# First batch of attention: the mask reads the scores in PSUM, against a threshold in the scores' own sign and scale

## The chip, the cores and the metric

The kernel runs on one core of a Trainium2 chip. The metric is the time of one execution on the device in microseconds, lower is better; the median of several runs counts. Everything is float32 (matmul operands are float32 split into a rounded high part and a low rest). Engines are named as in the profile: PE is TensorE (PEld its weight loads), DVE VectorE, ACT ScalarE, POOL GpSimd, SP the queue that issues most DMAs.

## The reference

Three stages follow one another. Attention keeps, in every row of scores, only those within `tau` of the row's maximum. Then come a gated two-layer block, and a block with a Fourier transform and an MLP.

```python
scores = scale * np.matmul(q, k.transpose(0, 1, 3, 2))      # scale = 1/sqrt(64), 4 batches x 8 heads, 576 x 576
thresh = np.max(scores, axis=-1, keepdims=True) - tau
scores = np.where(scores >= thresh, scores, -1000000000.0)
scores = scores - np.max(scores, axis=-1, keepdims=True)
attn = np.exp(scores)
attn = attn / (np.sum(attn, axis=-1, keepdims=True) + 1e-09)
out = np.matmul(attn, v)
...
xk = mu_k * x + (1.0 - mu_k) * x_prev                       # and xr with mu_r
k = np.maximum(xk @ w_k, 0.0)
v = k * k @ w_v
r = 1.0 / (1.0 + np.exp(-(xr @ w_r)))
x = r * v
...
u = x + np.real(np.fft.fft(np.fft.fft(x, axis=1), axis=2))
un = (u - mu) / np.sqrt(var + 1e-06)
ch = np.maximum(un @ w_ch1, 0.0) @ w_ch2
y = u + ch
```

## The kernel before

**Tiles.** Attention goes in tiles of 128 queries by all 576 keys. The heads of a batch are taken in pairs. A pair has nine tiles (`TILES_PAIR`): four of the first head, the tail tile (`TAIL`, the fifth, number 4 of the pair) that holds the last 64 queries of both heads, and four of the second head. A batch has four pairs, so 36 tiles (`TILES_BATCH`), and all four batches 144 (`TILES`). Tiles are numbered n = 0 to 143.

**The steps of a tile**, each on its engine:
- PE, `qk(n)` (L863): the scores into PSUM, two halves of 288 keys in two banks, by four matmuls (`k_hi` and `k_lo` for each half); a tail tile takes eight. In the first batch the tile has the two-bank tensor `PB[n % 2]`. From tile 36 on all tiles have `PB[0]`, since `PB[1]` then serves the dense stages.
- DVE, `row_max(n)` (L1414): reads the scores in PSUM, multiplies them by `taus[:, 2:3]` (minus the scale), writes the negated scaled scores to `neg_s` in SBUF, and gives their minimum, `negmax`. It announces `max_ready`.
- ACT, `exp(n)` (L1146, L1147): the threshold `negmax + |tau|`, a 128 x 1 operation, and `exps`, the exponential of the whole tile out of `neg_s`.
- DVE, `mask(n)` (L1429): `probs = (neg_s <= thresh) * exps` with the row's sum; in a tail tile one more operation for the last 64 keys (`both_last`, L1428). It announces `probs_ready`. After the tail tile and the last tile of a pair come two small operations for the inverse sums.
- PE, `transpose_probs(n)` (L881), four or five transposes in two units; ACT, `copy_units(n)` (L1156), copies the two units to `probsT`; PE, `pv(n)` (L901, L903), eight or nine pieces of the product with the values.
- ACT, `copy_tile` (L1174, L1177): the finished outputs, scaled, to `x_att`.

**The order** is written out by hand. Every engine walks over slots n = 0, 1, 2, ... and takes in slot n:
- PE: `qk(n)`, `transpose_probs(n-3)`, `pv(n-4)`, then dense work due in this slot.
- DVE: `row_max(n)`, `mask(n-1)`, then dense work.
- ACT: `exp(n)`, in slots 9 to 35 also a rounding of weights or tables (`weight_hi`), dense work, `copy_units(n-2)`, `copy_tile`.
- POOL: the low parts of the next keys and queries (`split_step`: L671, L685, L692) and of the weights and tables (L696 to L713), then dense work.

In the first batch there is no dense work yet. Dense work on a batch begins when its attention is done: in slot 38 for the first one. Semaphores order the engines; a buffer is given back by a semaphore too. The score buffer is given back for `qk(n)` by the wait that the change touches:

```python
if n >= TILES_BATCH:
    pe.wait_ge(max_ready, n)
elif n >= 2:
    pe.wait_ge(max_ready, n - 1)
```

so in the first batch `qk(n)` waits until the row maxima of tiles 0 to n-2 are done. `row_max(n)` for its part waits for `probs_ready` of tile n-2, since it overwrites the `neg_s` buffer that `mask(n-2)` read.

Of the kernel before, what the change touches and what calls it, by code (L numbers as in the profile page):

```python
# [22 lines left out]
F32 = mybir.dt.float32  # L23
F32R = mybir.dt.float32r
ALU = mybir.AluOpType
# [7 lines left out]
P128 = 128  # L33
# [35 lines left out]
EPS_SM = 1e-9  # L69

# [16 lines left out]
def place_of(n):  # L87


    return (2, 2, 1, 1, 0, 0, 0, 1, 1)[n % TILES_PAIR] * DH  # L90

# [140 lines left out]
def build(nc, qT, kT, v, tau, mu_k, mu_r, w_k, w_v, w_r, w_1, w_2, dft_d, dft_odd, dft_s, ident_in, cd_scr, odd_scr, cs_scr, u_scr, out):  # L232
    ctx = ExitStack()
    with ctx:
# [25 lines left out]
        taus = m.put("taus", [P128, 4], F32)  # L260
# [256 lines left out]
        with nc.Block() as block:  # L517
# [316 lines left out]
            def _(pe):  # L834
# [5 lines left out]
                def qk(n):  # L840
# [10 lines left out]
                    if n >= TILES_BATCH:  # L851

                        pe.wait_ge(max_ready, n)
                    elif n >= 2:
                        pe.wait_ge(max_ready, n - 1)
# [118 lines left out]
                def dense(d):  # L974

                    for dt in range(DT):
                        yield x_at(d, dt)
                        wait_evicted(d, "x", 0, dt)
                        if dt == 0 and d == 0:
                            pe.wait_ge(max_ready, TILES_BATCH)  # L980
# [158 lines left out]
            def _(act):  # L1139
                def exp(n):  # L1140
                    act.wait_ge(max_ready, n + 1)
                    if n >= 2:

                        act.wait_ge(probs_ready, n - 1)
                    col = n % (2 * TILES_PAIR)
                    nc.scalar.activation(thresh[:, col:col + 1], negmax[:, col:col + 1], ACT.Identity, bias=taus[:, 1:2]).then_inc(thr_ready, 1)  # L1146
                    nc.scalar.activation(exps[:, n % 2, :], neg_s[:, n % 2, :], ACT.Exp,  # L1147
                                         bias=negmax[:, col:col + 1], scale=-1.0).then_inc(exp_ready, 1)
# [202 lines left out]
                act.wait_ge(setup_b, 1)  # L1351
# [35 lines left out]
            def _(dve):  # L1387
# [16 lines left out]
                dve.wait_ge(setup_b, 1)  # L1404
                dve.wait_ge(pool_ready, 1)
# [11 lines left out]
                def mask(n):  # L1417
# [7 lines left out]
                    if jj == TAIL:  # L1425

                        twice = [t[:, n % 2, FULL * P128:S].unsqueeze(1).broadcast_to([P128, 2, DH]) for t in (neg_s, exps)]
                        nc.vector.scalar_tensor_tensor(both_last[:, :, :], twice[0], thresh[:, col:col + 1], twice[1], ALU.is_le, ALU.mult)  # L1428
                    nc.vector.scalar_tensor_tensor(probs[:, n % 2, place_of(n):place_of(n) + S], neg_s[:, n % 2, :], thresh[:, col:col + 1],  # L1429
                                                   exps[:, n % 2, :], ALU.is_le, ALU.mult,  # L1430
                                                   accum_out=rowsum[:, jj, 0:1]).then_inc(probs_ready, 1)
# [318 lines left out]
```

## Time and profile before

| | |
|---|---|
| runs, median | 1062.2 us (3 runs, 1061.6 to 1063.57) |
| the profiled execution, its own time | 1061.17 us |
| its span, first to last instruction | 1059.4 us |
| PE busy | 1032.3 us, 97% of the span |
| DVE busy | 584.9 us, 55% |
| ACT busy | 502.3 us, 47% |
| POOL busy | 415.4 us, 39% |
| granted TensorE clock, mean | 0.998 of full speed |

A busy share over the whole span is a mean over stages of different kinds: attention alone (about the first 100 us), attention beside dense work of the batch before, and the MLP at the end. So the tables by stretch of time and the timeline are read beside it. In a timeline row the bracket at the end tells how long the engine had stood idle before and who released it. An instruction that also writes an accumulator is followed by a row `DVE_READ_ACCUMULATOR`; its end is what others wait for.

### The profile page before, as it was taken

Reading aid. Unit: us, or ns where it says so; the run is one execution under the profiler, and the core shown is the slowest. Engines: PE = TensorE matmul, PEld = TensorE weight load, DVE = VectorE, ACT = ScalarE, POOL = GpSimd, SP = SyncE. Lnnn points to the kernel's source line nnn. Section 1 sums busy time; section 2 is a strip of 40 time slices with the busy share of each in tenths; the row PEclk is TensorE's granted clock in tenths of the full one; section 3 lists DMA queues with packets and bytes.
Section 4 is the critical chain, followed back from the end, with each engine's and each line's share of the span. In section 5 each row is a group of like instructions: output and inputs, shape, how many; then the busy total and the mean of one; then the engine's idle time right before and its main releaser. Section 6 shows DMA issues by size and latency. Waiting matters only on the chain.

```text
span 1059.4 us, 18202 instructions
## 1 busy us (share of the span) xinstructions
PE 1032.3 (97%) x6896; PEld 980.2 (93%) x6896; DVE 584.9 (55%) x1135; ACT 502.3 (47%) x1252; POOL 415.4 (39%) x363
## 2 busy tenths in 40 slices
PE   6999899999999999999999999999999999999998
PEld 5898899999999999999999999888888888888998
DVE  6998995467975477874565687443214214114111
ACT  5989785656775646775646643211111111111110
POOL 5878784333664434673423246331211211111000
PEclk9999999999999999999999999999999999999999
DMA  8736112033302032301023137101001100100000
GB/s 241 200 89 193 43 44 58 3 91 118 103 26 59 1 126 83 104 25 37 20 94 111 45 121 278 41 1 63 10 1 37 36 1 34 39 1 1 37 1 35
DMA packets 41271, 70.08 MB, mean 66 GB/s; under 512 B 6624, under 2 KB 22368, under 8 KB 40672
## 3 DMA queue, kind: packets, MB, share of 16 engines
q1 hardware_dynamic: 40880, 68.59, 20.6%
q8 instruction: 55, 0.90, 0.4%
q10 hardware_dynamic: 304, 0.33, 0.1%
q14 instruction: 32, 0.26, 0.1%
HBM read 56.50 MB, written 12.41 MB: 65 GB/s over the span
## 4 chain that ended last, share of the span: by engine, by line
PE 86%; DVE 4%; POOL 3%; ACT 3%; issue 3%; DMA 0%; SPq 0%; DVEq 0%; ACTq 0%; POOLq 0%
PE PB L836 22%; PE PB L837 21%; PE PB L838 21%; PE PB L901 8%; PE PB L863 6%; PE PB L881 5%; DVE probs L1429 2%; PE PB L903 1%; ACT probsT L1156 1%; ACT exps L1147 1%; PE PB L986 1%; DVE neg_s L1414 1%; POOL k_lo L692 0%; POOL q_hl L685 0%; POOL cs_lo L713 0%
## 5 line engine op out<-in xcount | busy, mean ns | idle before, releaser
L1373 ACT ACTIVATE h_hi<-PB 128x464 fp32r<-128x464 f32 (+1 forms) x80 | 44.4, 554 | 329.9 <-PE PB L838 329.9
L1652 DVE SCALAR_TENSOR_TENSOR h_lo<-PB,h_hi 128x464 fp32r<-128x464 f32 (+1 forms) x80 | 51.0, 637 | 256.7 <-ACT h_hi L1373 256.7
L1429 DVE SCALAR_TENSOR_TENSOR probs<-neg_s,thresh,exps 128x576 f32<-128x576 f32 x144 | 160.7, 1116 | 0.5 <-ACT exps L1147 0.2
L901 PE MATMUL PB<-v_sb,probsT 128*128 128x64 f32 (+1 forms) x1152 | 146.1, 270 | 0.0
L901 PEld LDWEIGHTS PB<-v_sb,probsT 128*128 128x128 f32 x1152 | 140.8, 193 | 0.0
L1414 DVE TENSOR_SCALAR_CACHE_REDUCE neg_s<-PB,taus 128x576 f32<-128x576 f32 x144 | 117.0, 812 | 40.2 <-PE PB L863 35.6
L1156 ACT ACTIVATE probsT<-PB 128x256 f32<-128x256 f32 (+1 forms) x288 | 103.6, 416 | 71.6 <-PE PB L881 70.8
L838 PE MATMUL PB<-un_h,w1l 128*128 128x464 f32 (+1 forms) x320 | 118.8, 371 | 0.0
L837 PE MATMUL PB<-h_lo,w2h 128*128 128x464 f32 (+1 forms) x320 | 118.8, 371 | 0.0
L836 PE MATMUL PB<-h_hi,w2h 128*128 128x464 f32 (+1 forms) x320 | 118.8, 371 | 0.0
L838 PE MATMUL PB<-h_hi,w2l 128*128 128x464 f32 (+1 forms) x320 | 118.8, 371 | 0.0
L836 PE MATMUL PB<-un_h,w1h 128*128 128x464 f32 (+1 forms) x320 | 118.7, 371 | 0.0
L837 PE MATMUL PB<-un_l,w1h 128*128 128x464 f32 (+1 forms) x320 | 118.6, 370 | 0.0
L1147 ACT ACTIVATE exps<-neg_s,negmax 128x576 f32<-128x576 f32 x144 | 112.5, 781 | 0.0
L735 POOL TENSOR_TENSOR mix_l<-mix_v,mix_h 128x288 fp32r<-128x288 f32 x64 | 55.4, 865 | 134.2 <-ACT mix_h L1234 133.7
L881 PE MATMUL PB<-ident,probs 128*128 128x128 f32 x640 | 94.7, 275 | 6.9 <-ACT probsT L1156 4.6
L881 PEld LDWEIGHTS PB<-ident,probs 128*128 128x128 f32 x640 | 76.4, 141 | 10.4 <-issue 6.6
L863 PE MATMUL PB<-k_hi,q_hl 128*128 128x288 f32 x320 | 74.6, 315 | 10.6 <-DVE q_hl L1395 6.8
L749 POOL TENSOR_TENSOR k_sql<-k_sq,k_sqh 128x288 fp32r<-128x288 f32 x56 | 48.9, 882 | 81.9 <-DVE k_sq L1529 81.9
L836 PE MATMUL PB<-k_sqh,wvh 128*128 128x288 f32 x256 | 78.4, 306 | 0.4 <-POOL k_sql L749 0.3
L836 PE MATMUL PB<-mix_h,wkh 128*128 128x288 f32 x256 | 78.2, 305 | 0.3 <-POOL mix_l L735 0.3
L837 PE MATMUL PB<-k_sql,wvh 128*128 128x288 f32 x256 | 76.3, 298 | 0.0
(204 smaller groups left out, 2431.4 us busy)
## 6 DMA issues: line engine op xcount, KB each, us to landing
q_raw<-qT_dram SPq DMA_DIRECT2D x62, 160.0 KB, 3.1
k_raw<-kT_dram SPq DMA_DIRECT2D x64, 144.0 KB, 3.2
w_raw<-w_dram SPq DMA_DIRECT2D x8, 1024.0 KB, 8.4
u_scr<-x2T SPq DMA_DIRECT2D x4, 1152.0 KB, 5.2
cd<-cd_scr SPq DMA_DIRECT2D x4, 1032.0 KB, 5.1
v_sb<-v_dram SPq DMA_DIRECT2D x16, 256.0 KB, 3.2
u_in<-u_scr SPq DMA_DIRECT2D x4, 928.0 KB, 5.1
out_dram<-u_in SPq DMA_DIRECT2D x16, 232.0 KB, 2.1
```

What stands on the lines that cost most here:

```text
L735: nc.gpsimd.tensor_tensor(mix_l[kind][:, dt, :], mix_v[:, i % 2, :], mix_h[kind][:, dt, :].bitcast(F32), ALU.subtract).then_inc(mixl_ready, 1)
L836: nc.tensor.matmul(o, ah, rh, start=start, stop=False)
L837: nc.tensor.matmul(o, ah, rl, start=False, stop=False)
L838: return nc.tensor.matmul(o, al, rh, start=False, stop=stop)
L863: last = nc.tensor.matmul(scores(n)[:, half, :], q_hl[:, h, i * P128:(i + 1) * P128], kk[:, h, half * HALF:half * HALF + HALF], start=h == ...
L881: last = nc.tensor.transpose(bank(4 + unit % 2)[:, (kt - k0) * P128:(kt - k0 + 1) * P128], keys, ident[:, :])
L901: last = nc.tensor.matmul(both[:, own], probsT[:, n % 2, kt * P128:(kt + 1) * P128], v_sb[:, kt, pair % 2, own], start=jj in (0, TAIL) and ...
L1147: nc.scalar.activation(exps[:, n % 2, :], neg_s[:, n % 2, :], ACT.Exp, bias=negmax[:, col:col + 1], scale=-1.0).then_inc(exp_ready, 1)
L1156: nc.scalar.activation(probsT[:, n % 2, k0 * P128:k1 * P128], bank(4 + unit % 2)[:, 0:(k1 - k0) * P128], ACT.Copy).then_inc(unit_copied, 1)
L1414: nc.vector.tensor_scalar(neg_s[:, n % 2, :].rearrange("p (a n) -> p a n", a=2), scores(n), taus[:, 2:3], None, ALU.mult, ALU.min, accum_o ...
L1429: nc.vector.scalar_tensor_tensor(probs[:, n % 2, place_of(n):place_of(n) + S], neg_s[:, n % 2, :], thresh[:, col:col + 1], exps[:, n % 2, ...
L1652: nc.vector.scalar_tensor_tensor(h_lo[:, ft % 3, 0:w], bank(4 + ft % 3)[:, 0:w], 0.0, h_hi[:, ft % 3, 0:w].bitcast(F32), ALU.max, ALU.subt ...
```

## The change

Tiles of the first batch (`from_psum(n)`, n < 36) are masked out of PSUM. Their mask compares the raw scores in `PB` with a threshold of the raw scores, by `is_ge` in place of `is_le`. `row_max` stays as it is and `neg_s` is still written and is read by `exps`. ACT computes the threshold with a scale of -8 and another bias, `taus[:, 4:5]`, which two more small DVE operations prepare at the start. The score buffer is given back by `probs_ready` in place of `max_ready`: for `qk(n)` with n from 2 to 36, and for the first transposes of `x_att` that use `PB[1]`.

```diff
--- before.py
+++ after.py
@@ -67,6 +67,7 @@
 
 EPS_LN = 1e-6
 EPS_SM = 1e-9
+LOWEST = 2.0 ** 124
 
 
 def rows_of(i):
@@ -88,6 +89,11 @@
 
 
     return (2, 2, 1, 1, 0, 0, 0, 1, 1)[n % TILES_PAIR] * DH
+
+
+def from_psum(n):
+
+    return n < TILES_BATCH
 
 
 def units_of(n):
@@ -257,7 +263,7 @@
         at_y_h2 = m.at
         m.at += 2 * HALF * 4
         y_h2 = Place(at_y_h2).put("y_h2", [P128, 2 * KC], F32R)
-        taus = m.put("taus", [P128, 4], F32)
+        taus = m.put("taus", [P128, 8], F32)
         mus = m.put("mus", [P128, 2, DT], F32)
         omus = m.put("omus", [P128, 2, DT], F32)
         negmax = m.put("negmax", [P128, 2 * TILES_PAIR], F32)
@@ -848,11 +854,11 @@
                     if jj == TAIL:
 
                         pe.wait_ge(qk_split, pair * 2 + 2)
-                    if n >= TILES_BATCH:
+                    if n > TILES_BATCH:
 
                         pe.wait_ge(max_ready, n)
                     elif n >= 2:
-                        pe.wait_ge(max_ready, n - 1)
+                        pe.wait_ge(probs_ready, n - 1)
                     i = row_of(n)
                     heads = (0, 1) if jj == TAIL else (p,)
                     for h in heads:
@@ -977,7 +983,7 @@
                         yield x_at(d, dt)
                         wait_evicted(d, "x", 0, dt)
                         if dt == 0 and d == 0:
-                            pe.wait_ge(max_ready, TILES_BATCH)
+                            pe.wait_ge(probs_ready, TILES_BATCH)
                         if dt == 0 and alone(d):
 
                             pe.wait_ge(max_ready, TILES)
@@ -1143,7 +1149,11 @@
 
                         act.wait_ge(probs_ready, n - 1)
                     col = n % (2 * TILES_PAIR)
-                    nc.scalar.activation(thresh[:, col:col + 1], negmax[:, col:col + 1], ACT.Identity, bias=taus[:, 1:2]).then_inc(thr_ready, 1)
+                    if from_psum(n):
+
+                        nc.scalar.activation(thresh[:, col:col + 1], negmax[:, col:col + 1], ACT.Identity, bias=taus[:, 4:5], scale=-(DH ** 0.5)).then_inc(thr_ready, 1)
+                    else:
+                        nc.scalar.activation(thresh[:, col:col + 1], negmax[:, col:col + 1], ACT.Identity, bias=taus[:, 1:2]).then_inc(thr_ready, 1)
                     nc.scalar.activation(exps[:, n % 2, :], neg_s[:, n % 2, :], ACT.Exp,
                                          bias=negmax[:, col:col + 1], scale=-1.0).then_inc(exp_ready, 1)
 
@@ -1348,7 +1358,7 @@
                 act.wait_ge(qk_in[0], 64)
                 for cols in (slice(0, P128), slice(P128, SQ)):
                     nc.scalar.activation(q_hl[:, 0, cols], q_raw[:, 0, cols], ACT.Copy).then_inc(head0_q_hi, 1)
-                act.wait_ge(setup_b, 1)
+                act.wait_ge(setup_b, 3)
                 beside = [[Beside(mixing(d)), Beside(dense(d))] for d in range(B)]
                 for n in range(SLOTS):
                     if n < TILES:
@@ -1402,6 +1412,10 @@
                 dve.wait_ge(setup_a, 1)
                 nc.vector.tensor_tensor(taus[:, 1:2], taus[:, 0:1], taus[:, 3:4], ALU.max).then_inc(setup_b, 1)
                 dve.wait_ge(setup_b, 1)
+
+                nc.vector.tensor_scalar(taus[:, 5:6], taus[:, 2:3], -(DH ** 0.5) * LOWEST, -LOWEST, ALU.mult, ALU.add).then_inc(setup_b, 1)
+                dve.wait_ge(setup_b, 2)
+                nc.vector.scalar_tensor_tensor(taus[:, 4:5], taus[:, 1:2], -(DH ** 0.5), taus[:, 5:6], ALU.mult, ALU.add).then_inc(setup_b, 1)
                 dve.wait_ge(pool_ready, 1)
 
                 def row_max(n):
@@ -1422,13 +1436,20 @@
                     if n >= 2:
 
                         dve.wait_ge(unit_ready, 2 * n - 2)
-                    if jj == TAIL:
-
-                        twice = [t[:, n % 2, FULL * P128:S].unsqueeze(1).broadcast_to([P128, 2, DH]) for t in (neg_s, exps)]
-                        nc.vector.scalar_tensor_tensor(both_last[:, :, :], twice[0], thresh[:, col:col + 1], twice[1], ALU.is_le, ALU.mult)
-                    nc.vector.scalar_tensor_tensor(probs[:, n % 2, place_of(n):place_of(n) + S], neg_s[:, n % 2, :], thresh[:, col:col + 1],
-                                                   exps[:, n % 2, :], ALU.is_le, ALU.mult,
-                                                   accum_out=rowsum[:, jj, 0:1]).then_inc(probs_ready, 1)
+                    last_keys = [t.unsqueeze(1).broadcast_to([P128, 2, DH]) for t in (scores(n)[:, 1, FULL * P128 - HALF:HALF], neg_s[:, n % 2, FULL * P128:S], exps[:, n % 2, FULL * P128:S])]
+                    place = probs[:, n % 2, place_of(n):place_of(n) + S]
+                    if from_psum(n):
+                        if jj == TAIL:
+
+                            nc.vector.scalar_tensor_tensor(both_last[:, :, :], last_keys[0], thresh[:, col:col + 1], last_keys[2], ALU.is_ge, ALU.mult)
+                        nc.vector.scalar_tensor_tensor(place.rearrange("p (a n) -> p a n", a=2), scores(n), thresh[:, col:col + 1],
+                                                       exps[:, n % 2, :].rearrange("p (a n) -> p a n", a=2), ALU.is_ge, ALU.mult,
+                                                       accum_out=rowsum[:, jj, 0:1]).then_inc(probs_ready, 1)
+                    else:
+                        if jj == TAIL:
+                            nc.vector.scalar_tensor_tensor(both_last[:, :, :], last_keys[1], thresh[:, col:col + 1], last_keys[2], ALU.is_le, ALU.mult)
+                        nc.vector.scalar_tensor_tensor(place, neg_s[:, n % 2, :], thresh[:, col:col + 1], exps[:, n % 2, :], ALU.is_le, ALU.mult,
+                                                       accum_out=rowsum[:, jj, 0:1]).then_inc(probs_ready, 1)
                     if jj in (TAIL, TILES_PAIR - 1):
                         head = pair * 2 + p
                         tiles = slice(p * QT, TILES_PAIR if p else QT)
```

How the instructions stand, first on PE, in slot 5 and the start of slot 6: the scores of tile 5 into `PB1`, the transposes of tile 2 (`PB2`), the values of tile 1 (`PB3`), the scores of tile 6. Before:

```order
L863 MATMUL PB1<-k_hi_70,q_hl_69 128x288 [waits max_ready]
L863 MATMUL PB1<-k_hi_70,q_hl_69 128x288
L863 MATMUL PB1<-k_lo_71,q_hl_69 128x288 x2
L881 MATMUL PB2<-ident_49,probs_73 128x128 [waits unit_copied,probs_ready]
L881 MATMUL PB2<-ident_49,probs_73 128x128
L881 MATMUL PB2<-ident_49,probs_73 128x128 [waits unit_copied]
L881 MATMUL PB2<-ident_49,probs_73 128x128
L901 MATMUL PB3<-v_sb_72,probsT_75 128x64 [waits unit_copied]
L901 MATMUL PB3<-v_sb_72,probsT_75 128x64 x3
L863 MATMUL PB0<-k_hi_70,q_hl_69 128x288 [waits max_ready]
```

After:

```order
L869 MATMUL PB1<-k_hi_70,q_hl_69 128x288 [waits probs_ready]
L869 MATMUL PB1<-k_hi_70,q_hl_69 128x288
L869 MATMUL PB1<-k_lo_71,q_hl_69 128x288 x2
L887 MATMUL PB2<-ident_49,probs_73 128x128 [waits unit_copied,probs_ready]
L887 MATMUL PB2<-ident_49,probs_73 128x128
L887 MATMUL PB2<-ident_49,probs_73 128x128 [waits unit_copied]
L887 MATMUL PB2<-ident_49,probs_73 128x128
L907 MATMUL PB3<-v_sb_72,probsT_75 128x64 [waits unit_copied]
L907 MATMUL PB3<-v_sb_72,probsT_75 128x64 x3
L869 MATMUL PB0<-k_hi_70,q_hl_69 128x288 [waits probs_ready]
```

The order is the same; the score matmuls now wait for `probs_ready`, the mask, where they waited for `max_ready`, the row maximum.

On DVE, from the row maximum of tile 3 to the mask of the tail tile, 4. Before:

```order
L1414 TENSOR_SCALAR neg_s_78,negmax_54<-PB1,taus_51 128x576 [waits probs_ready,scores_ready]
L1429 SCALAR_TENSOR_TENSOR probs_73,rowsum_56<-neg_s_78,thresh_55,exps_77 128x576 [waits unit_ready,thr_ready,exp_ready]
L1414 TENSOR_SCALAR neg_s_78,negmax_54<-PB0,taus_51 128x576 [waits probs_ready,scores_ready]
L1429 SCALAR_TENSOR_TENSOR probs_73,rowsum_56<-neg_s_78,thresh_55,exps_77 128x576 [waits unit_ready,thr_ready,exp_ready]
L1414 TENSOR_SCALAR neg_s_78,negmax_54<-PB1,taus_51 128x576 [waits probs_ready,scores_ready]
L1428 SCALAR_TENSOR_TENSOR both_last_74<-neg_s_78,thresh_55,exps_77 128x128 [waits unit_ready,thr_ready,exp_ready]
L1429 SCALAR_TENSOR_TENSOR probs_73,rowsum_56<-neg_s_78,thresh_55,exps_77 128x576
```

After, with two rows more ahead of them for `taus`:

```order
L1428 TENSOR_SCALAR neg_s_78,negmax_54<-PB1,taus_51 128x576 [waits probs_ready,scores_ready]
L1445 SCALAR_TENSOR_TENSOR probs_73,rowsum_56<-PB0,thresh_55,exps_77 128x576 [waits unit_ready,thr_ready,exp_ready]
L1428 TENSOR_SCALAR neg_s_78,negmax_54<-PB0,taus_51 128x576 [waits probs_ready,scores_ready]
L1445 SCALAR_TENSOR_TENSOR probs_73,rowsum_56<-PB1,thresh_55,exps_77 128x576 [waits unit_ready,thr_ready,exp_ready]
L1428 TENSOR_SCALAR neg_s_78,negmax_54<-PB1,taus_51 128x576 [waits probs_ready,scores_ready]
L1444 SCALAR_TENSOR_TENSOR both_last_74<-PB0,thresh_55,exps_77 128x128 [waits unit_ready,thr_ready,exp_ready]
L1445 SCALAR_TENSOR_TENSOR probs_73,rowsum_56<-PB0,thresh_55,exps_77 128x576
```

The order is again the same; the masks' first operand is `PB0` or `PB1` (PSUM) where it was `neg_s_78` (SBUF). `row_max(n)` stands directly behind `mask(n-2)`.

## Rows read from the trace of the kernel before

**Rows 1.** The page, busy us, share of the span, instructions.
```profile
PE 1032.3 (97%) x6896; PEld 980.2 (93%) x6896; DVE 584.9 (55%) x1135; ACT 502.3 (47%) x1252; POOL 415.4 (39%) x363
```

**Rows 2.** Windows: length, busy us of PE, PEld, DVE, ACT, POOL, PEclk, DMA.
```profile
28.27:60.71 32.44, 29.80 (x248) 28.43 (x247) 30.05 (x64) 31.45 (x81) 22.93 (x19) 1.00 0.70 195
60.71:91.44 30.73, 27.89 (x231) 26.53 (x230) 28.27 (x60) 27.20 (x78) 29.05 (x20) 1.00 0.50 149
116.95:150.00 33.05, 33.05 (x268) 32.91 (x267) 30.09 (x49) 27.16 (x75) 27.65 (x24) 1.00 0.17 46
```

**Rows 3.** Timeline (start us, us, engine): row maxima of tiles 2, 9, 23, 36.
```profile
12.82 0.82 DVE L1414 TENSOR_SCALAR_CACHE_REDUCE neg_s<-PB,taus 128x576 f32<-128x576 f32 x1
...
28.27 0.82 DVE L1414 TENSOR_SCALAR_CACHE_REDUCE neg_s<-PB,taus 128x576 f32<-128x576 f32 x1
...
60.71 0.82 DVE L1414 TENSOR_SCALAR_CACHE_REDUCE neg_s<-PB,taus 128x576 f32<-128x576 f32 x1
...
91.44 0.82 DVE L1414 TENSOR_SCALAR_CACHE_REDUCE neg_s<-PB,taus 128x576 f32<-128x576 f32 x1 [0.15 <-PE PB L863]
```

**Rows 4.** Groups on DVE, 8 to 91 us: busy, mean ns, idle before.
```profile
L1429 DVE SCALAR_TENSOR_TENSOR probs<-neg_s,thresh,exps 128x576 f32<-128x576 f32 x35 | 43.2, 1235 | 0.5 <-ACT exps L1147 0.2
L1414 DVE TENSOR_SCALAR_CACHE_REDUCE neg_s<-PB,taus 128x576 f32<-128x576 f32 x36 | 29.4, 817 | 5.9 <-PE PB L863 2.7
```

**Rows 5.** Timeline of DVE and POOL, 66 to 74 us.
```profile
66.46 0.81 DVE L1429 SCALAR_TENSOR_TENSOR probs<-neg_s,thresh,exps 128x576 f32<-128x576 f32 x1
67.19 0.08 DVE L1429 DVE_READ_ACCUMULATOR probs<-neg_s,thresh,exps 128x1 f32 x1
...
71.49 1.56 POOL L685 TENSOR_TENSOR q_hl<-q_raw,q_hl 64x640 fp32r<-64x640 f32 x1
71.70 1.97 DVE L1429 SCALAR_TENSOR_TENSOR probs<-neg_s,thresh,exps 128x576 f32<-128x576 f32 x1
```

**Rows 6.** Two tiles on DVE: duration ns min/median/max, first and last start.
```profile
L1558 DVE TENSOR_TENSOR x2T<-PB,gate x28: 440/456/458, 161.2 to 612.7; 128x288 f32<-128x288 f32 x28
L1529 DVE TENSOR_TENSOR k_sq<-k_relu x64: 395/458/1806, 138.2 to 627.2; 128x288 f32<-128x288 f32 x64
```

**Rows 7.** Timeline of PE: first score matmuls of tiles 36 and 37.
```profile
90.64 0.50 PE L863 MATMUL PB<-k_hi,q_hl 128*128 128x288 f32 x2
...
92.82 0.51 PE L863 MATMUL PB<-k_hi,q_hl 128*128 128x288 f32 x2
```

**Rows 8.** Timeline: scores of tile 40 (a tail tile), and scores of tile 43.
```profile
100.81 0.53 PE L863 MATMUL PB<-k_hi,q_hl 128*128 128x288 f32 x2 [0.41 <-POOL k_lo L692]
...
102.18 0.82 DVE L1414 TENSOR_SCALAR_CACHE_REDUCE neg_s<-PB,taus 128x576 f32<-128x576 f32 x1 [0.36 <-PE PB L863]
...
111.14 0.08 DVE L1414 DVE_READ_ACCUMULATOR neg_s<-PB,taus 128x1 f32 x1
111.27 0.53 PE L863 MATMUL PB<-k_hi,q_hl 128*128 128x288 f32 x2 [1.21 <-DVE neg_s L1414]
111.64 0.42 PE L863 MATMUL PB<-k_lo,q_hl 128*128 128x288 f32 x2
```

**Rows 9.** Timeline of DVE: both_last and mask of tail tile 40.
```profile
107.55 0.34 DVE L1428 SCALAR_TENSOR_TENSOR both_last<-neg_s,thresh,exps 128x128 f32<-128x128 f32 x1
107.81 0.81 DVE L1429 SCALAR_TENSOR_TENSOR probs<-neg_s,thresh,exps 128x576 f32<-128x576 f32 x1
```

**Rows 10.** Timeline: scores and row maximum of tile 1, mask of tile 0.
```profile
8.93 0.85 PE L863 MATMUL PB<-k_hi,q_hl 128*128 128x288 f32 x2 [0.59 <-POOL q_hl L666]
...
10.30 0.82 DVE L1414 TENSOR_SCALAR_CACHE_REDUCE neg_s<-PB,taus 128x576 f32<-128x576 f32 x1 [0.96 <-PE PB L863]
...
11.04 1.64 DVE L1429 SCALAR_TENSOR_TENSOR probs<-neg_s,thresh,exps 128x576 f32<-128x576 f32 x1
```

**Rows 11.** Timeline of PE: two more waits between 100 and 116 us.
```profile
107.03 0.63 PE L986 MATMUL PB<-ident,x_att 128*128 128x128 f32 x4 [1.38 <-ACT x_att L1177]
...
114.75 0.53 PE L863 MATMUL PB<-k_hi,q_hl 128*128 128x288 f32 x2 [1.30 <-DVE neg_s L1414]
```

## The prediction

> **What bounds the kernel now.** Start with the page [rows 1]: TensorE is busy 97% of the span, so nothing but TensorE's idle time can be won or lost, and the question is where that idle time lies. The table of windows [rows 2] answers it. From 116.95 us on TensorE has no gap (33.05 us busy in a window of 33.05), and whatever moves that point moves the end by as much. Before it lies the first batch, the only stretch the change touches: TensorE is busy 29.80 of 32.44 us and 27.89 of 30.73, VectorE 30.05 and 28.27. There is no dense work beside attention yet, and VectorE sets the pace with two big instructions per tile.
>
> Next, the pace. VectorE's row maxima (L1414) mark the tiles. Tile 2's starts at 12.82, tile 9's at 28.27, tile 23's at 60.71, tile 36's (the first of batch 1) at 91.44 [rows 3]. That is 78.62 us for 34 tiles, 2.31 us each. The groups of this stretch [rows 4] say what fills it: a row maximum takes 817 ns, always the same, a mask (L1429) 1235 ns in the mean. The timeline [rows 5] shows why the mask varies: alone it takes 0.81 us; the one that starts at 71.70, just after GpSimd began a two-input operation at 71.49, takes 1.97. The two engines keep each other out, and the mask pays (1.235 - 0.81) x 35 = 15 us of VectorE time for that in the first batch.
>
> **What the change takes away.** The mask (and `both_last` in the tail tile) reads its scores in PSUM, so one SBUF tensor is left as input. Rows of that form stand in the trace [rows 6]: x2T<-PB,gate reads PSUM and SBUF 28 times between 161 and 613 us, with GpSimd at work in much of it, and never takes more than 458 ns; k_sq<-k_relu, with both inputs in SBUF and the same size, has the same median and a maximum of 1806. So I take each of the 36 masks at the 0.81 of the undisturbed one, and GpSimd's operations lose their waits too. The Trainium skill (SBUF — State Buffer, "Who interferes with whom") says the same in general, that a VectorE instruction with at most one SBUF input does not contend with GpSimd. The bounds for one mask are 0.76 (VectorE's 464-column operation with a PSUM input stands on the page at 637 ns; at 1.04 ns a column that is 754 for 576) and 1.24 (nothing gained). I take 0.81 since the row maximum, which reads the same 576 columns out of PSUM, takes 0.82 [rows 4].
>
> **What the change adds.** The price is a wait. Score buffers alternate between two halves of PSUM. Before, the score matmuls (QK) of tile n waited for the row maximum of tile n-2; now they wait for its mask. On VectorE the order is row max n-1, mask n-2, row max n. Row max n is therefore next in line behind the very mask that QK(n) waits for, and QK(n) must run before it. Before, QK(n) ran under mask n-2; now VectorE stands still while it runs, in every tile. The chain closes into a loop:
> - mask n-2, its start to the end of its accumulator read: 0.82.
> - to the first QK matmul: 0.05. From [rows 8]: the accumulator read that starts at 111.14 ends at 111.22, and the waiting QK starts at 111.27.
> - QK start to row max start: 0.83. In [rows 8] such a QK ends at 111.64 + 0.42 = 112.06, 0.79 after its start; row maxima start about 0.04 after the scores ([rows 7] and [rows 3]: 90.64 to 91.44 is 0.80, with the weights already loaded).
> - row max start to mask n-1 start: 0.74 ([rows 5] have that step for the mask, 66.46 to 67.19; the row max has it too).
>
> The sum is 2.44 us per tile. A tail tile (4, 13, 22, 31) has eight matmuls instead of four, 1.37 instead of 0.83 ([rows 8], 100.81 to 102.18, 0.54 more; I take 0.56), and `both_last`, 0.26 when undisturbed [rows 9]: 0.82 more each.
>
> What else must fit under 2.44? TensorE's own slot is 2.19 (QK to QK, [rows 7]) even with five transposes and nine value matmuls, so it waits about 0.25 per tile and is not the bound. Behind the waiting QK stand the transposes of tile n-3 and the values of n-4; they start 0.6 after QK, and the mask that needs the transposed buffer free comes 1.57 after it, so that still fits. ScalarE gets `exps` done in the 2.4 us between row max n and mask n. Its worst stretch is tiles 9 to 23 with the weight roundings: 31.45 us of work [rows 2] against 14 x 2.44 + 2 x 0.82 = 35.8, enough in the sum but uneven in tiles 12 to 16. I add 0.5 (0 to 1.5). GpSimd has the longer time and the shorter operations. The two small operations on `taus` at the start fit into VectorE's wait for the first scores and cost nothing; were that cover gone, 0.3. The new scale of the threshold costs nothing. The reductions after every tail and last tile now lie in VectorE's gap.
>
> **The sum.** Tile 2 to tile 36: 34 x 2.44 + 4 x 0.82 = 86.2 against 78.62, so +7.6. The start: mask 0 begins at 11.04 [rows 10], ends at 11.86, QK(2) starts at 11.91, and this early a QK takes 1.37 (its first pair of matmuls 0.85 against 0.53 later, [rows 10], [rows 8]), so row max 2 starts at 13.28 instead of 12.82: +0.5. With the new gaps the slow matmuls may last two tiles longer: +0.5 (0 to 1.6). ScalarE +0.5. Coming back: in tile 40 QK waited 0.41 for GpSimd's k_lo [rows 8]; GpSimd will be far ahead, so -0.4. From tile 36 on everything has the old form and TensorE's own pace, so the shift stays: +8.7 us. On the profiled execution (1061.17, span 1059.4) that is 1069.9; the median of the runs, 1062.2, lies 1.0 above it, so I say 1070.9.
>
> **A page against the rows.** x2T from PSUM has a median of 456 ns, k_sq from SBUF 458 [rows 6]: no price for the source. The Trainium skill (VectorE: DVE Perf Modes, the errata-adjusted cycle table) gives a PSUM source 120 fixed cycles against 58. By that page, as an estimate, 62 cycles at its 0.96 GHz are 65 ns a mask, in the loop every time, and the sum would be 2.3 us more.
>
> **Rivals.**
> - *The delay is absorbed late.* Between 100 and 115 us TensorE stands idle four times: 0.41, 1.38, 1.21, 1.30, together 4.3 [rows 8, 11]. If GpSimd's lead and emptier queues cure all of them, 8.7 + 0.4 - 4.3 = +4.8: 1067.0. Against it: the 1.38 is a chain through ScalarE's x_att copies of tile 40 that starts with QK(40), and moves with it. Chance 0.13.
> - *PSUM source dearer.* If the mask from PSUM costs some 0.06 more than the row of equal size shows, the loop is 2.50: +10.8, 1073.1. This is what the cycle table above makes of it. The median of x2T speaks against it. Chance 0.05.
> - *The collision stays* (the change does not do what it says). If the mask keeps its 1.235 us in the loop, 0.42 x 34 = 14 more: 1085. The maximum of 458 for x2T speaks against it. Chance 0.04.
> - *Faster: the wait never binds.* If TensorE reaches QK(n) later than the end of mask n-2, since ScalarE and its own slots (1.9 to 2.2) hold it back, the loop does not close and only the freed 15 us of collisions count. Tiles 2 to 9 would go at about 1.9 and tiles 23 to 36 at 2.1, while tiles 9 to 23 stay with ScalarE: 2.1 and 3.4 us gained, 5.6 in all: 1056.6. The point from which it decides: TensorE's slot must be longer than the loop, 2.44. The longest regular slot in the trace is 2.19. Chance 0.06.
> - *Nothing to be seen.* The loop at 2.25 or less, between these, or a short loop and full absorption together: within 2 us of before. Chance 0.06.
>
> **How the numbers follow.** The forecast has 0.66. Its own range comes from the loop at 2.38 or 2.49 (34 x 0.06 = 2.0 down, 1.7 up), the slow start and ScalarE at zero (-1.0) or at their ends (+2.1): 1067.5 to 1075. The range of 8 in 10 also takes in late absorption with room below: 1065.5 to 1075, which leaves out the faster and equal cases, the lasting collision and a little on both ends. A measurement of this kernel can tell about 0.2%, 2.1 us, from no change. Slower: 0.66 + 0.13 + 0.05 + 0.04 = 0.88; same 0.06; faster 0.06.
>
> **What would show it.** In the profile after: masks of the first 36 tiles at 0.81 with no long ones; VectorE idle about 0.85 us before each row max there, released by TensorE (L863's new line), some 25 to 30 us in all where 2.7 stood [rows 4]; TensorE waiting for the mask before QK some 0.25 us a tile; row max of tile 36 near 99.5; the point of full TensorE near 125. I am wrong if the row max of tile 36 comes before 96 (the loop does not bind) or after 103 (mask or ScalarE dearer), or if it comes at 99.5 and TensorE is full before 122 (late absorption).

## The result and the profile after

The changed kernel takes 1072.1 us (median of 4 runs, 1071.56 to 1072.89) against 1061.9 before: ratio 1.0095, 95% interval 1.008 to 1.011, so 10.2 us slower. Its profiled execution has a span of 1070.3 us.

The lines of VectorE in the first batch, 8 to 104 us, as groups (busy us, mean ns, idle before and its releaser); they answer to [rows 4]:

```profile
L1428 DVE TENSOR_SCALAR_CACHE_REDUCE neg_s<-PB,taus 128x576 f32<-128x576 f32 x37 | 30.2, 817 | 33.3 <-PE PB L869 33.3
L1445 DVE SCALAR_TENSOR_TENSOR probs<-PB,thresh,exps 128x576 f32<-128x576 f32 x35 | 28.5, 813 | 0.7 <-issue 0.4
```

The masks went from 1235 to 813 ns in the mean. VectorE's waits for the scores went from 2.7 to 33.3 us. The next lines are one turn of the loop in the changed kernel's timeline, to be held against [rows 5] and [rows 8]:

```profile
52.73 0.82 DVE L1428 TENSOR_SCALAR_CACHE_REDUCE neg_s<-PB,taus 128x576 f32<-128x576 f32 x1 [0.88 <-PE PB L869]
...
53.47 0.81 DVE L1445 SCALAR_TENSOR_TENSOR probs<-PB,thresh,exps 128x576 f32<-128x576 f32 x1
54.21 0.08 DVE L1445 DVE_READ_ACCUMULATOR probs<-PB,thresh,exps 128x1 f32 x1
...
54.34 0.54 PE L869 MATMUL PB<-k_hi,q_hl 128*128 128x288 f32 x2 [0.27 <-DVE probs L1445]
54.72 0.42 PE L869 MATMUL PB<-k_lo,q_hl 128*128 128x288 f32 x2
...
55.19 0.82 DVE L1428 TENSOR_SCALAR_CACHE_REDUCE neg_s<-PB,taus 128x576 f32<-128x576 f32 x1 [0.90 <-PE PB L869]
```

Read it as steps: row max to mask 0.74, mask to the end of its accumulator read 0.82, 0.05 to the first score matmul, 0.85 to the next row max: 2.46. Of the 34 steps from tile 2 to tile 36, 19 are 2.44 to 2.46 and 3 more at most 2.52. The row maxima of tiles 2, 6 and 36, and the windows of the start and of the batch (columns as in [rows 2]):

```profile
13.67 0.82 DVE L1428 TENSOR_SCALAR_CACHE_REDUCE neg_s<-PB,taus 128x576 f32<-128x576 f32 x1 [1.42 <-PE PB L869]
...
26.82 0.82 DVE L1428 TENSOR_SCALAR_CACHE_REDUCE neg_s<-PB,taus 128x576 f32<-128x576 f32 x1 [0.47 <-PE PB L869]
...
103.91 0.82 DVE L1428 TENSOR_SCALAR_CACHE_REDUCE neg_s<-PB,taus 128x576 f32<-128x576 f32 x1 [0.96 <-PE PB L869]
```

```profile
0.00:24.00 24.00, 11.80 (x45) 10.16 (x46) 10.39 (x28) 8.42 (x18) 9.72 (x15) 1.00 0.83 215
24.00:104.00 80.00, 72.03 (x561) 67.18 (x560) 52.18 (x144) 67.53 (x176) 51.41 (x45) 1.00 0.55 162
104.00:128.00 24.00, 20.12 (x171) 19.50 (x170) 19.34 (x46) 19.06 (x53) 12.37 (x12) 1.00 0.17 45
128.00:150.00 22.00, 22.00 (x179) 21.86 (x179) 19.58 (x32) 18.70 (x52) 17.69 (x15) 1.00 0.25 72
```

VectorE is no longer full (52 of 80 us), and no other engine is either (TensorE 72, ScalarE 68): a loop of waits sets the pace. The row max of tile 36 comes 12.47 us later than before (103.91 against 91.44, [rows 3]), that of tile 43 11.78 later, and TensorE's last wait up to 150 us ends at 126.52 instead of 114.75 [rows 11].

### The profile page after: what moved, and what is told of

Read it like the earlier page. It is cut to its first block, busy times and chain, and to the rows that moved or that the text cites. A ratio compares the mean times of both kernels' runs of the same rounds, so it can differ in the third digit from the quotient of the medians.

```text
span 1070.3 us, 18204 instructions
## 1 busy us (share of the span) xinstructions
PE 1038.0 (97%) x6896; PEld 983.5 (92%) x6896; DVE 570.0 (53%) x1137; ACT 503.1 (47%) x1252; POOL 402.2 (38%) x363
## 4 chain that ended last, share of the span: by engine, by line
PE 90%; DVE 4%; ACT 3%; issue 2%; POOL 1%; DMA 0%; SPq 0%; ACTq 0%; DVEq 0%; POOLq 0%
PE PB L842 21%; PE PB L843 21%; PE PB L844 21%; PE PB L907 9%; PE PB L869 9%; PE PB L887 6%; PE PB L909 2%; DVE probs L1445 1%; DVE neg_s L1428 1%; PE PB L992 1%; ACT x_att L1187 1%; DMA k_raw<-kT_dram 0%; ACT exps L1157 0%; ACT probsT L1166 0%; ACT mix_v L1229 0%
## 5 line engine op out<-in xcount | busy, mean ns | idle before, releaser
L1451 DVE SCALAR_TENSOR_TENSOR probs<-neg_s,thresh,exps 128x576 f32<-128x576 f32 x108 | 117.5, 1088 | 0.0
L869 PEld LDWEIGHTS PB<-k_hi,q_hl 128*128 128x128 f32 x320 | 51.5, 194 | 31.0 <-DVE probs L1445 14.4
```

The lines of the kernel that those rows point to most:

```text
L869: last = nc.tensor.matmul(scores(n)[:, half, :], q_hl[:, h, i * P128:(i + 1) * P128], kk[:, h, half * HALF:half * HALF + HALF], start=h == ...
L1451: nc.vector.scalar_tensor_tensor(place, neg_s[:, n % 2, :], thresh[:, col:col + 1], exps[:, n % 2, :], ALU.is_le, ALU.mult, accum_out=rows ...
```

## The experiments

A note for reading: "before" was run beside each set again; its median lay between 1061.3 and 1062.8. Ratios are to the kernel before on the same chip. Where row maxima are given, they are those of the profiled execution.

**The wait alone.** Only the semaphores of the change, with the mask on `neg_s` in SBUF:

```diff
-                    if n >= TILES_BATCH:
+                    if n > TILES_BATCH:
...
-                        pe.wait_ge(max_ready, n - 1)
+                        pe.wait_ge(probs_ready, n - 1)
...
-                            pe.wait_ge(max_ready, TILES_BATCH)
+                            pe.wait_ge(probs_ready, TILES_BATCH)
```

> The kernel before with one part of the change alone: the score matmuls of the first batch wait for the mask of tile n-2 instead of its row maximum; the mask still reads neg_s in SBUF. Theory of the loop (the wait is what costs): the loop closes here too, 2.45 us a tile, and the collisions of the mask with GpSimd stay inside it, some 0.3 us a tile in the mean, 34 x 0.3 = 10 us more than with the change: 1082 (1077 to 1087). Rival (reading PSUM, or the threshold, is what costs and the wait hardly matters): within 2 us of before, 1060 to 1064.

Measured: 1096.5 us, ratio 1.0336 (1.032 to 1.0352). The rival is out: the wait costs 35 us by itself, and reading PSUM wins 24 of them back. The size was missed by 14 us, outside the stated range. The two groups (8 to 128 us) and the window of its first batch:

```profile
L1429 DVE SCALAR_TENSOR_TENSOR probs<-neg_s,thresh,exps 128x576 f32<-128x576 f32 x36 | 44.7, 1242 | 1.5 <-PE PB L881 1.0
L1414 DVE TENSOR_SCALAR_CACHE_REDUCE neg_s<-PB,taus 128x576 f32<-128x576 f32 x37 | 30.3, 818 | 38.4 <-PE PB L863 38.4
```

```profile
14.00:127.00 113.00, 87.77 (x590) 82.85 (x590) 75.96 (x155) 72.77 (x186) 61.26 (x49) 0.91 0.47 139
```

The expectation had put the mean mask at 1.1 us; it is 1242 ns, which makes 0.42 x 34 = 14 us more than in the changed kernel, and with `both_last` (1139 ns in the mean) some 18. And the granted clock is 0.91 in this stretch, where it was 1.00 in the changed kernel. It falls to the lower of TensorE's two levels (0.50 in the window, 1.2 GHz) for a while and comes back. One place of it, with the window behind it:

```profile
51.05 0.53 PE L863 MATMUL PB<-k_hi,q_hl 128*128 128x288 f32 x2 [0.91 <-DVE probs L1429]
...
55.85 0.85 PE L863 MATMUL PB<-k_hi,q_hl 128*128 128x288 f32 x2 [2.73 <-DVE probs L1429]
```

```profile
55.50:60.00 4.50, 4.15 (x18) 4.13 (x19) 2.31 (x8) 2.39 (x6) 0.00 (x0) 0.50 0.89 252
```

A pair of score matmuls takes 0.53 us, and 0.85 after the wait of 2.73; score matmuls stand in the loop, so each such tile is longer again. The row max of tile 36 comes at 127.2. How many of the 35 us are the clock was not measured.

**Freedom from collisions alone.** The waits of before, and a mask with a single SBUF tensor. It leaves out the comparison, so its output is not the reference's (the old mask stays for the later tiles):

```diff
-                    nc.vector.scalar_tensor_tensor(probs[...], neg_s[:, n % 2, :], thresh[:, col:col + 1], exps[:, n % 2, :], ALU.is_le, ALU.mult, accum_out=...)
+                    if n < TILES_BATCH:
+                        nc.vector.tensor_scalar(place, exps[:, n % 2, :], thresh[:, col:col + 1], None, ALU.max, ALU.add, accum_out=...)
...
```

> The kernel before, with its waits, but in the first batch the mask is an operation with a single SBUF tensor as input (the maximum of exps and the threshold, summed): the comparison is left out, so what is computed is not the reference; the tail tile's both_last stays as it was. It shows what freedom from collisions is worth without the wait. Theory: masks at 0.81 us, the batch goes on at the pace of TensorE and ScalarE, about 2.15 us a tile, 5 to 6 us faster than before: 1056 (1054 to 1058.5). Rival (the collisions lie beside other work and cost nothing): 1060 to 1063.

Measured: 1054.7 us, ratio 0.9941 (0.9928 to 0.9955), as expected. Its groups, 8 to 86 us:

```profile
L1414 DVE TENSOR_SCALAR_CACHE_REDUCE neg_s<-PB,taus 128x576 f32<-128x576 f32 x37 | 30.3, 818 | 12.9 <-PE PB L863 11.5
L1431 DVE TENSOR_SCALAR_CACHE_REDUCE probs<-exps,thresh 128x576 f32<-128x576 f32 x35 | 28.3, 809 | 1.3 <-ACT exps L1147 1.3
```

With the kernels before and after this fills a table (medians, us):

| | scores wait for the row max | scores wait for the mask |
|---|---|---|
| mask with two SBUF inputs | 1061.5 | 1096.5 |
| mask with one SBUF input | 1054.7 | 1072.1 |

The wait costs 35.0 where masks collide and 17.4 where they don't; one SBUF input is worth 6.9 without the wait and 24.4 with it. The change as a whole is +10.6 in this table and +10.2 beside its own runs of before (1061.9). The kernel behind 1054.7 has another operation as its mask and keeps `both_last` on two SBUF inputs, so the second row compares like with like only roughly.

**Is the start dearer?** The change for tiles 6 to 35 only (`from_psum` is `n >= 6` besides; a score buffer is given back by the mask only where its tile is masked out of PSUM).

> The change for tiles 6 to 35 only; tiles 0 to 5 are masked out of SBUF with the old wait. Theory (the start costs more per tile than the rest, since TensorE's gaps keep its first matmuls slow until about 23 us): the 4.9 us that tile 6 is late in the changed kernel nearly vanish, 0.5 remain at the seam: 1067.7 (1066 to 1069). Rival (every tile pays the same): 6/36 of 10 us, 1070.4.

Measured: 1067.4 us, ratio 1.0058 (1.0043 to 1.0074), as expected. The first six tiles are 4.7 of the 10.2 us by the medians, 4.3 by the row max of tile 43 (121.38 against 125.66). In this kernel the row max of tile 6 comes at 22.36 (21.95 before, 26.82 in the changed kernel). At the seam it pays something back: behind a wait of 1.99 us its granted clock is 0.50 from 28 to 30 us, and the steps to tiles 9 and 10 take 3.39 and 2.77 where the changed kernel has 2.86 and 2.44.

**Is it the score matmuls in the loop?** `k_lo` left out in tiles 2 to 35, in both kernels:

```diff
-                        for step, kk in enumerate((k_hi, k_lo)):
+                        for step, kk in enumerate((k_hi,) if 2 <= n < TILES_BATCH else (k_hi, k_lo)):
```

> The changed kernel with the k_lo matmuls of tiles 2 to 35 left out (two of four score matmuls, four of eight in a tail tile), so the scores are less exact than the reference's. Theory of the loop: the score matmuls stand in the loop, each tile shrinks by their 0.27 us, 2.45 to 2.18, a tail tile by 0.53: 34 x 0.27 + 4 x 0.27 = 10 us, and some 1 us at the slow start: 1061 (1059.5 to 1063). Rival (another engine paces the changed kernel, the score matmuls run beside it): 1069 to 1072.

> The same omission in the kernel before. Theory: there the score matmuls run under the masks, and only where TensorE or the scores were late for the row maximum does it help: 1 to 3 us, 1059.5 (1058 to 1061). Rival (the score matmuls are worth the same in both kernels): 1051.5.

Measured: in the changed kernel 1066.1 us, 6.0 less than the change, ratio to before 1.0046 (1.0031 to 1.0061); in the kernel before 1061.7, ratio 1.0005 (0.9989 to 1.0022), nothing. So the score matmuls are in the path of the one and not of the other, and the rivals of both fall. The steps show it to the size: 16 of the 34 are 2.18 to 2.21 where they were 2.44 to 2.46. Both totals lie above their stated ranges, though: the first wins 6 us where 10 in the loop and 1 at the start were expected, the second nothing where 1 to 3 were. The windows of the changed kernel with this omission:

```profile
24.00:88.00 64.00, 56.06 (x435) 51.49 (x435) 45.49 (x124) 57.84 (x156) 43.99 (x39) 1.00 0.54 160
88.00:98.00 10.00, 9.27 (x53) 9.10 (x52) 5.50 (x15) 7.40 (x18) 7.44 (x7) 0.66 0.98 266
```

From 88 to 98 us the granted clock is 0.66: here too TensorE fell to its lower level late in the batch, and its last two steps took 3.25 and 3.66 us, 2.5 more than the loop gives for them; most of the rest of the gap is in the steps to tiles 15, 22, 33 and 34. The kernel before with the same omission has such a fall as well: 0.61 from 44 to 48 us and 0.54 from 48 to 52, where before had 1.00 all through, and its row max of tile 36 comes at 94.60 instead of 91.44. So a gain of a few us from the omission may be hidden there. What sets off the falls was not looked into.

**The change where masks collide most.** Four tail tiles only.

> The change for the four tail tiles only (4, 13, 22, 31), whose masks, two operations, collide with GpSimd most (1.3 to 2.2 us, and 0.5 to 1.5 for both_last). Theory: each such tile pays the wait of 0.73 once and saves 1.5 in its own collisions, part of which moves to the neighbours: 1 to 3 us faster than before, 1060 (1058.5 to 1061.5). Rival (collisions only move to the next mask, the wait stays): 4 x 0.73 = 3 us slower, 1065.

Measured: 1062.0 us, ratio 1.001 (0.9999 to 1.0021): neither theory; no change. On the spot it works (the row max of tile 6 comes 1.1 us earlier than before, that of tile 24 2.0), but by tile 27 it is 1.0 late. After the tail tile 22 GpSimd's next long operations meet two of the three masks behind it (tiles 23 and 25), which before had taken 0.81 and 0.89 us:

```profile
64.27 1.28 POOL L715 TENSOR_TENSOR cd_lo<-cd_raw,cd_hi 128x516 fp32r<-128x516 f32 x1
...
64.45 1.71 DVE L1451 SCALAR_TENSOR_TENSOR probs<-neg_s,thresh,exps 128x576 f32<-128x576 f32 x1
...
69.89 1.93 DVE L1451 SCALAR_TENSOR_TENSOR probs<-neg_s,thresh,exps 128x576 f32<-128x576 f32 x1
69.91 1.29 POOL L715 TENSOR_TENSOR cd_lo<-cd_raw,cd_hi 128x516 fp32r<-128x516 f32 x1
```

**Opening the loop by another order.** Tiles 0 to 35 two by two, in the form for VectorE, TensorE and ScalarE:

```diff
+                    if n < TILES_BATCH and n % 2 == 0:
+                        row_max(n)
+                        row_max(n + 1)
+                        mask(n)
+                        mask(n + 1)
...
+                for n in range(0, TILES_BATCH, 2):
+                    qk(n)
+                    if n >= 2:
+                        transpose_probs(n - 2)
+                    qk(n + 1)
+                    if n >= 4:
+                        pv(n - 4)
+                        pv(n - 3)
+                    if n >= 2:
+                        transpose_probs(n - 1)
...
+                for n in range(0, TILES_BATCH, 2):
+                    exp(n)
+                    if n >= 2:
+                        copy_units(n - 2)
+                    exp(n + 1)
+                    if n >= 2:
+                        copy_units(n - 1)
```

> The changed kernel with tiles 0 to 35 taken two by two: VectorE does row max n, row max n+1, mask n, mask n+1; TensorE scores n, transposes n-2, scores n+1, values n-4 and n-3, transposes n-1; ScalarE exps n, copies n-2, exps n+1, copies n-1. rowinv has two halves, and the last of the small taus operations reads one SBUF tensor. Masks read PSUM as in the change. Theory: the row maximum no longer stands right behind the mask its scores wait for, the loop opens, and the batch goes at the pace of TensorE and ScalarE, 2.1 to 2.25 us a tile, as where the collisions were gone without the wait (1054.7): 1056 (1053.5 to 1060). Rival (the wait costs its 0.87 us of VectorE wherever it stands): above 1066.

Measured: 1064.7 us, ratio 1.0027 (1.0018 to 1.0036). That lies between the theory and its rival, outside both: the order takes back 7 of the 10 us, but the batch does not reach 2.15 us a tile (81.0 for 34 tiles is 2.38). Its waits from 10 to 95 us (us, times, longest):

```profile
ACT thresh L1164 <- DVE neg_s L1455: 12.4, 11, 2.7
DVE probs L1472 <- ACT exps L1167: 11.2, 15, 1.5
...
DVE neg_s L1455 <- PE PB L869: 5.2, 11, 1.0
```

VectorE's wait for scores fell from 33.3 to 5.2 us, and a new one stands in its place: 11.2 us for `exps`, while ScalarE waits 12.4 us for the row max. Each waits for the other in turn, which looks like the latency of a chain; that was argued from the waits, and no run took the chain apart.

**Is it ScalarE's load?** The thresholds of two tiles as one 128 x 2 operation on VectorE; then also the roundings of `w_k` in other slots; that move alone in the kernel before; and the last form with masks out of SBUF.

```diff
+                        dve.wait_ge(max_ready, n + 2)
+                        nc.vector.tensor_scalar(thresh[:, two], negmax[:, two], -(DH ** 0.5), taus[:, 4:5], ALU.mult, ALU.add).then_inc(thr_ready, 2)
...
+WK_HI_AT = (14, 16, 23, 25)
```

> The kernel with tiles taken in pairs (masks out of PSUM), and the thresholds of the first batch computed on VectorE, one 128 x 2 operation per pair, in place of two on ScalarE. In the kernel in pairs ScalarE was busy 28.7 of 30 us from 30 to 60 and the masks waited 11 us for exps. Theory (with the loop open ScalarE sets the pace): 0.2 us of ScalarE less per tile, of which some 24 tiles feel it, 3 to 5 us off 1064.7: 1060.5 (1059 to 1062.5). Rival (the waits for exps are a latency from row maximum to mask, not load): the threshold's latency moves to VectorE and nothing is gained, 1063.5 to 1066.

> The same, and ScalarE's four roundings of w_k moved from slots 13 to 16 to slots 14, 16, 23 and 25, where it has no other rounding. Theory of ScalarE's load: its peak goes, 1 to 2 us more: 1059 (1057 to 1061.5). Rival as above: no change to the kernel without the move.

> The kernel before with the roundings of w_k moved in the same way and nothing else, so that this move is not credited to the rest. In tiles 9 to 23 ScalarE was busy 31.45 of 32.44 us. Expected: 0 to 1.5 us faster than before, 1060.7 (1059.5 to 1062).

> The kernel in pairs with thresholds on VectorE and the roundings moved, but the masks read neg_s in SBUF and the scores wait for the row maximum as before: PSUM taken out of the best form. Theory: masks at 1.2 us again; VectorE has room (20 of 30 us busy in pairs), but a longer mask also delays the next exps and transposes, so 2 to 5 us more than with PSUM masks: 1063 (1061 to 1065). Rival (once in pairs, the collisions are hidden and the earlier release of the score buffers helps): equal to or below the PSUM form, 1057 to 1060.

Measured: 1069.2 us, ratio 1.0062 (1.0045 to 1.0079); with the roundings moved 1066.2, ratio 1.0039 (1.0025 to 1.0053); the roundings alone 1061.2 against 1062.8, ratio 0.9984 (0.9975 to 0.9994); masks out of SBUF 1083.7, ratio 1.0191 (1.0171 to 1.0211). Only the third came as expected. The first two had been put at 1060.5 and 1059, and the first lies beyond its rival's range too; the last had been put at 1063 and missed by 21 us. The theory of load is not borne out: with less on ScalarE the kernel in pairs became slower. The small operation is probably part of why, since it was anything but small (one line, min/median/max ns):

```profile
L1686 DVE TENSOR_SCALAR thresh<-negmax,taus x18: 228/604/1392, 11.2 to 96.2; 128x2 f32<-128x2 f32 x18
```

Two elements a partition, and up to 1.4 us. The 5 of them that met no GpSimd operation took 0.23 us each, the 13 that met one 0.38 to 1.39. Whether load would have counted with a cheap threshold was therefore not answered. Moving the roundings is worth 1.6 us in the kernel before, and some 3 in pairs (the intervals of the two overlap, so that size is loose). The last kernel says that in pairs, too, PSUM masks are worth 17 us, even with the earlier release of the score buffers given up for them; the rival, that collisions would be hidden there, is out. Its clock also fell (0.87 to 0.94 in windows of 30 us from 30 to 120), and I did not part the two shares.

**Picking two tiles.**

> The kernel before with the roundings of w_k moved (0.16% faster alone), and the change for two tiles only, 4 and 22, where the kernel with all four tail tiles changed was 1.1 and 2.0 us ahead of before shortly after. Theory: a mask out of PSUM wins where it takes away a collision of over 1 us and costs one wait of 0.73; of 3 us won on the spot most is waited for again by ScalarE and GpSimd, 0.5 to 1 us stay: 1060.3 against 1061.9 before (1059 to 1061.5). Rival (as with all four tails, nothing stays, and the wait is left over): 1061 to 1063.

Measured: 1060.3 us against 1062.05, ratio 0.9982 (0.9971 to 0.9993). The time is the expected one, but it is also what the roundings alone give (0.9984), so nothing that could be measured is left of the two PSUM masks. Both kernels beat before and after, by 0.2%, and the credit goes to the roundings.

## Why the prediction was right, point by point

- **Bound and place.** Right. What the batch lost reached the end: 12.47 us at tile 36, 11.78 at tile 43, and the row maxima keep that distance within 0.1 us up to tile 114. There the kernel before loses 0.8 us: in its profiled execution the granted clock is 0.62 for 4 us near 420 while TensorE is busy. The spans differ by 10.9 us, the medians by 10.2.
- **What is taken away.** Right: 813 ns for each mask, none long, and no price for PSUM as a source. The estimate of 65 ns more per mask, worked out from the Trainium skill (VectorE: DVE Perf Modes, errata-adjusted cycle table), did not show: 813 against 0.81 us [rows 5].
- **The loop.** 2.44 us forecast, 2.44 to 2.46 measured. The experiments with the wait alone and with half the score matmuls show that it is this wait and these matmuls.
- **The start: mis-sized.** For the slow matmuls behind tile 2 the forecast had 0.5 (0 to 1.6). From tile 2 to tile 6 the loop gives 4 x 2.44 + 0.82 = 10.58; it took 13.15, so 2.6 more, outside the stated bounds. The pairs of score matmuls of tiles 2 to 4 took 0.82 to 0.85 us, and came down to 0.53 only at tile 6, where in the kernel before they were at 0.54 from tile 4 on; the eight matmuls of tail tile 4 made one step of 4.22. The profile's clock column shows 1.00 there all the same, so the slow start is read from the matmuls. Changed kernel, then before:

```profile
18.58 0.82 PE L869 MATMUL PB<-k_hi,q_hl 128*128 128x288 f32 x2 [1.11 <-DVE probs L1445]
...
25.98 0.53 PE L869 MATMUL PB<-k_hi,q_hl 128*128 128x288 f32 x2 [0.64 <-DVE probs L1445]
```

```profile
13.99 0.54 PE L863 MATMUL PB<-k_hi,q_hl 128*128 128x288 f32 x2 [0.27 <-POOL k_lo L692]
```

- **"The two small operations cost nothing".** Right, though it doesn't look so. The last of them took 0.98 us for a single element a partition, beside GpSimd's first long operation, and pushed row max 0 back by 0.3 us. Row max 1 still had to wait for its scores. That it began at 10.69 instead of 10.30 has another reason: in the changed kernel's profiled execution the first keys arrived 0.38 us later, ahead of the added operations. The kernel of the tail tiles has the same two operations and its row max 1 at 10.33. So 0.4 of the 12.47 and 11.78 us is this arrival and not the change. The changed kernel, the kernel before, the kernel of the tail tiles:

```profile
6.25 0.46 DVE L1403 CAST k_hi<-k_raw 128x576 fp32r<-128x576 f32 x1 [5.03 <-DMA k_raw<-kT_dram]
...
8.00 1.26 POOL L672 TENSOR_TENSOR q_hl<-q_raw,q_hl 64x512 fp32r<-64x512 f32 x1 [6.23 <-DVE k_lo L1407]
...
8.30 0.98 DVE L1418 SCALAR_TENSOR_TENSOR taus<-taus 128x1 f32<-128x1 f32 x1
```

```profile
5.87 0.46 DVE L1393 CAST k_hi<-k_raw 128x576 fp32r<-128x576 f32 x1 [4.65 <-DMA k_raw<-kT_dram]
```

```profile
10.33 0.82 DVE L1428 TENSOR_SCALAR_CACHE_REDUCE neg_s<-PB,taus 128x576 f32<-128x576 f32 x1 [0.67 <-PE PB L869]
```

- **ScalarE.** 0.5 forecast (0 to 1.5). Tiles 6 to 36 took 77.09 against 30 x 2.44 + 3 x 0.82 = 75.66, so 1.4 more, but little of it can be put down to ScalarE. The loop's 0.01 to 0.02 more per tile, the tail tiles and the steps to tiles 18, 27 and 36 take about 0.6. The steps to tiles 9 and 28 are 0.42 and 0.26 longer than the loop; in them VectorE stood idle for 0.24 and 0.18 before a mask, and the trace names no engine that it waited for. In the step to tile 15 the reductions behind the tail tile waited for ScalarE's copies to `x_att` and ended 0.15 after the row max was due: in this place they did not fit into VectorE's gap.
- **Coming back.** 0.4 forecast, 0.69 measured. The three waits that the rival of late absorption wanted to see vanish stayed to within 0.01, as the chain of `x_att` had it ([rows 8, 11]: 1.38, 1.21, 1.30):

```profile
118.82 0.63 PE L992 MATMUL PB<-ident,x_att 128*128 128x128 f32 x4 [1.38 <-ACT x_att L1187]
123.05 0.53 PE L869 MATMUL PB<-k_hi,q_hl 128*128 128x288 f32 x2 [1.21 <-DVE neg_s L1428]
126.52 0.53 PE L869 MATMUL PB<-k_hi,q_hl 128*128 128x288 f32 x2 [1.29 <-DVE neg_s L1428]
```

- **The sum, and some luck.** 8.7 forecast, 10.2 measured by the medians (8.5 to 11.7). By the traces the parts were further off: 11.8 at tile 43, of which the start makes up 2.1 more than forecast, the batch behind tile 6 0.9, the late arrival 0.4, and the coming back 0.3 less. The total stands nearer the forecast than its parts, in the profiled pair through the 0.8 us that the kernel before lost at its fall of the clock, which has nothing to do with the change. My own signs for being wrong would have fired, too: I had written "after 103" for the row max of tile 36, and it came at 103.9. The "near 99.5" beside it was not my own sum, which gives 91.44 + 9.1 = 100.5; the two halves for the start and ScalarE were left out of it. The lower end of my own range is also 0.4 below what its terms give (1067.9).
- **The rival on the other side.** Its price was about right (1056.6; the kernel with one input and the old wait gave 1054.7), its condition was not met, as [rows 7] had said (2.18 from score matmuls to score matmuls).

## What to carry to other kernels

A buffer's release moved from its first reader to its second is not a small wait: look at what stands next on the second reader's engine. If that is the consumer of what the release lets in, the producer's whole time, hidden until then, enters every step. Work out the loop step by step from start to start; here it came out to 1%. The edges of a stage, where the pipe fills and TensorE has gaps, need a sum of their own. Removing contention from an operation is worth most where that operation has just been put into such a loop, and such a gain is not a reason for the loop. And before a shift of some tenths between two traces is put down to an edit, look whether it stands there already ahead of the changed instructions.

## What the runs showed of the hardware

- A VectorE operation that GpSimd holds back is not protected by being short. One element a partition out of two SBUF inputs took 0.98 us beside a GpSimd operation; the kernel in pairs, where that operation reads one SBUF tensor, has it at 0.21 beside the same GpSimd operation. Yet two elements out of one SBUF tensor, in the first kernel with thresholds on VectorE, took 0.38 to 1.39 us wherever they met GpSimd, and 0.23 elsewhere. So a few bytes of bookkeeping on VectorE beside a busy GpSimd can be a long operation. The Trainium skill (SBUF — State Buffer, "Who interferes with whom") says that VectorE with two SBUF inputs contends with a GpSimd instruction that reads SBUF, and that `tensor_scalar` can contend in its two-port modes; the runs agree with the first, and whether the second is what held the two elements back no run here shows. The line of 0.98 stands above; that of 0.21:

```profile
8.15 1.26 POOL L672 TENSOR_TENSOR q_hl<-q_raw,q_hl 64x512 fp32r<-64x512 f32 x1 [6.38 <-DVE k_lo L1434]
...
8.45 0.21 DVE L1445 TENSOR_SCALAR taus<-taus 128x1 f32<-128x1 f32 x1
```

- Collisions did not thin out when the pace slowed: 1235 ns mean at 2.31 us a tile, 1242 at 3.3 us a tile in the kernel with the wait alone. That GpSimd's work is set off by TensorE's progress, and so comes at the same places of the pattern, would explain it; that was not tested.
- A loop of waits can cost twice: with TensorE busy 88 of 113 us and single waits up to 2.7 us the granted clock averaged 0.91, and 0.66 over 10 us in another kernel. In the changed kernel, with gaps of some 0.25 us a tile and 90% busy from 24 to 104 us, it stayed at 1.00.
